# Dense stage: the next block's rows turned by VectorE in squares of 32 in place of TensorE's transposes

## The reference

```python
def _moe2_ref(x, w_in, w_out):        # x 4352 x 512, w_in 512 x 2048, w_out 2048 x 512
    h = x @ w_in
    neg = h <= -1.0
    pos = h >= 1.0
    g = np.where(pos, h, np.where(neg, 0.0, (h + 1.0) ** 2 / 4.0))
    return (g @ w_out).astype(np.float32)
```

## Time and profile before

| | |
|---|---|
| median of 3 runs | 1357.77 us (1357.71 to 1357.79) |
| the profiled execution's own time | 1359.21 us |
| its span, first to last instruction | 1357.5 us |
| mean granted TensorE clock | 0.995 |
| TensorE matmuls busy | 1333.6 us (98%) |
| VectorE busy | 776.6 us (57%) |
| ScalarE busy | 406.3 us (30%) |
| dense stage, first hidden to last result | 583.2 to 1345.2 us |

### The profile page before, as it was taken

How to read it: one execution, slowest core, us unless ns; L and a number is a source line. 1 busy time by engine, 2 the same in 40 slices (tenths; PEclk the granted TensorE clock), 3 DMA queues, 4 the chain that set the end, 5 groups by cost and what they waited for, 6 DMA issues and landing times.

```text
span 1357.5 us, 19931 instructions
## 1 busy us (share of the span) xinstructions
PE 1333.6 (98%) x6638; PEld 1116.2 (82%) x6639; DVE 776.6 (57%) x1521; ACT 406.3 (30%) x641; POOL 386.6 (28%) x213
## 2 busy tenths in 40 slices
PE   8999999999999999999999999999999999999996
PEld 6998888888888888788888888888888888888885
DVE  4677888888888888754444444444444444444342
ACT  3555222222222222322222222222222222222232
POOL 2377372775571849270010100100001001010010
PEclk9999999999999999999999999999999999999998
DMA  6656233434441525420010100100100001010000
GB/s 151 170 167 222 107 110 106 170 108 142 136 170 46 169 78 191 136 94 16 16 40 17 38 16 16 39 15 8 47 15 34 18 9 39 15 39 1 0 32 16
DMA packets 80586, 100.54 MB, mean 74 GB/s; under 512 B 46112, under 2 KB 46112, under 8 KB 80032
## 3 DMA queue, kind: packets, MB, share of 16 engines
q1 hardware_dynamic: 60160, 61.94, 14.9%
q10 hardware_dynamic: 13856, 20.19, 4.8%
q0 software_dynamic: 6528, 17.87, 3.5%
HBM read 69.80 MB, written 30.18 MB: 74 GB/s over the span
## 4 chain that ended last, share of the span: by engine, by line
PE 94%; DMA 1%; DVE 1%; issue 1%; POOL 0%; ACT 0%; ACTq 0%; SPq 0%; POOLq 0%; DVEq 0%
PE area L1685 27%; PE area L1699 27%; PE area L1635 15%; PE area L1593 14%; PE area L1403 2%; PE area L1373 2%; PE area L1527 1%; PE area L1393 1%; PE area L1671 1%; PE area L1360 1%; DMA xin<-in_x 1%; PE area L1420 1%; PE area L1427 0%; DMA st_diag<-in_state 0%; DMA slot_x<-rows,found 0%
## 5 line engine op out<-in xcount | busy, mean ns | idle before, releaser
L1699 PE MATMUL area<-W,gs 128*128 128x512 f32 x1632 | 397.4, 391 | 1.0 <-DVE gs L1267 1.0
L1685 PE MATMUL area<-ys,W 128*128 128x512 f32 (+1 forms) x1728 | 394.4, 377 | 0.0
L1685 PEld LDWEIGHTS area<-ys,W 128*128 128x128 f32 x1728 | 313.4, 188 | 61.2
L1699 PEld LDWEIGHTS area<-W,gs 128*128 128x128 f32 x1632 | 303.0, 188 | 62.7 <-DVE gs L1267 1.4
L1213 DVE STREAM_TRANSPOSE area<-hrow 32x256 f32<-32x256 f32 x592 | 269.9, 456 | 75.3 <-ACT hrow L718 66.3
L600 POOL DMA_INDIRECT out<-orow,out_row x34 | 32.7, 961 | 708.4 <-ACT orow L804 618.5
L788 ACT ACTIVATE gate<-gate,half_col 128x512 f32<-128x512 f32 (+1 forms) x144 | 100.7, 700 | 440.7 <-DVE gate L1262 439.6
L1262 DVE TENSOR_SCALAR gate<-area 128x512 f32<-128x512 f32 (+1 forms) x144 | 95.3, 662 | 224.3 <-PE area L1685 224.1
L1635 PE MATMUL area<-W,hs 128*128 (+1 forms) x912 | 218.9, 396 | 0.5 <-issue 0.3
L1593 PE MATMUL area<-W,xs 128*128 x864 | 202.0, 389 | 0.2 <-issue 0.2
L1635 PEld LDWEIGHTS area<-W,hs 128*128 128x128 f32 x912 | 169.6, 189 | 35.5 <-issue 1.1
(11 more groups left out here) (195 smaller groups left out, 799.1 us busy)
## 6 DMA issues: line engine op xcount, KB each, us to landing
stage<-in_moe_w SPq DMA_DIRECT2D x32, 1024.0 KB, 5.5
sorted_y<-ytile ACTq DMA_DIRECT2D x38, 256.0 KB, 2.1
xtile<-slot_x ACTq DMA_DIRECT2D x36, 256.0 KB, 2.7
yrow<-sorted_y SPq DMA_DIRECT2D x34, 256.0 KB, 2.6
xin<-in_x SPq DMA_DIRECT2D x60, 128.0 KB, 2.9
stage<-in_moe_w_in SPq DMA_DIRECT2D x4, 1024.0 KB, 4.9
stage<-in_moe_w_out SPq DMA_DIRECT2D x4, 1024.0 KB, 5.3
slot_x<-zero SPq DMA_DIRECT2D x9, 256.0 KB, 3.2
```

The costliest lines, as they stand in the source:

```text
L1685: last = nc.tensor.matmul(HIDDEN[n % 2][:, 0:width], wq[:, wp, :], ys[par][:, yp, k, 0:width], start=(k == 0 and wp == HI and yp == HI), s ...
L1699: last = nc.tensor.matmul(SUMS[a], gs[n % 2][:, gp, a * P:(a + 1) * P], W[:, q // 2 + 2, wp, at:at + DM], start=(n == 0 and gp == HI and w ...
```

## The change

The transposes of TensorE in the dense stage's loop go (both calls of `turn_next` in it). VectorE turns each of the 30 row tiles in 16 instructions, each four squares of 32 (32 partitions by 128 elements), from `yrow` to the same PSUM banks. They are spread over three slices n, in pairs: behind the clamp (part 0), behind the maximum (part 1) and behind the low part (part 2). For a row tile with turning slice T the pairs stand at n = T - 2 (parts 1 and 2), T - 1 (all parts) and T (all parts); `yt_made` rises at the end of n = T. `weigh` moves from behind n = T - 2 to behind the low part of n = T - 3, and `y_lo` from behind n = T to behind the clamp of n = T + 1. The turning slices of block 0 become 5, 8, 11, 14. The turning of the first four row tiles, and ScalarE's and SyncE's programs, are as before but for those slices.

```diff
-        FIRST_TURN_AT = (6, 9, 12, 14)
+        FIRST_TURN_AT = (5, 8, 11, 14)
...
+            def squares(j, k, first, end):
+
+                if first == 0:
+                    dve.wait_ge(weighted, j + 1)
+                    dve.wait_ge(ylo_done, j - 1)
+                turned = TURNED[k].rearrange("p (d s) -> p d s", d=KD)
+                for r, q in ((n // 4, n % 4) for n in range(first, end)):
+                    last = nc.vector.transpose(
+                        turned[SQ * q:SQ * (q + 1), :, SQ * r:SQ * (r + 1)],
+                        yrow[k][SQ * r:SQ * (r + 1), :].rearrange("p (d f) -> p d f", d=KD)[:, :, SQ * q:SQ * (q + 1)])
+                if end == 16:
+                    last.then_inc(yt_made, 1)
+
+            def turn_beside(i, n, part, par, turned, turn_at):
+
+                for a in range(turned):
+                    j, at = first_row(i + 1) + a, n - turn_at[a] + 2
+                    if at == 3 and part == 0:
+                        y_lo(j, 1 - par, a)
+                    if at == 0 and part > 0:
+                        squares(j, a % 2, 2 * part - 2, 2 * part)
+                    if at in (1, 2):
+                        squares(j, a % 2, 6 * at - 2 + 2 * part, 6 * at + 2 * part)
+                for a in range(turned):
+                    if part == 2 and n == turn_at[a] - 3:
+                        weigh(first_row(i + 1) + a, a % 2)
+
-            def gates(i, n, width):
+            def gates(i, n, width, par, turned=BIG, turn_at=TURN_AT):
                 h, g = HIDDEN[n % 2][:, 0:width], gate[n % 2][:, 0:width]
                 dve.wait_ge(hidden_made, K2 * i + n + 1)
                 nc.vector.tensor_scalar(g, h, -1.0, 1.0, ALU.max, ALU.min).then_inc(clamped, 1)
-
+                turn_beside(i, n, 0, par, turned, turn_at)
                 dve.wait_ge(squared, K2 * i + n + 1)
                 nc.vector.tensor_tensor(h, g, h, ALU.max).then_inc(gated, 1)
+                turn_beside(i, n, 1, par, turned, turn_at)
                 dve.wait_ge(ghi_done, K2 * i + n + 1)
                 nc.vector.tensor_tensor(gs[n % 2][:, LO, 0:width], h, gs[n % 2][:, HI, 0:width].bitcast(F32), ALU.subtract
                                         ).then_inc(glo_done, 1)
+                turn_beside(i, n, 2, par, turned, turn_at)
...
-            def turns(i, n, par, turned=BIG, turn_at=TURN_AT):
-                if n + 2 in turn_at[:turned]:
-                    a = turn_at.index(n + 2)
-                    weigh(first_row(i + 1) + a, a % 2)
-                if n in turn_at[:turned]:
-                    a = turn_at.index(n)
-                    y_lo(first_row(i + 1) + a, 1 - par, a)
...
             def block_of_rows(i, par, next_width=BIG * P):
                 for n in range(1, K2):
                     hidden(i, par, n)
-                    if n in TURN_AT[:next_width // P]:
-                        turn_next(i, TURN_AT.index(n))
                     result(i, n - 1)
...
-                if n in FIRST_TURN_AT:
-                    turn_next(0, FIRST_TURN_AT.index(n))
```

More of the change, by code:

```diff
@@ L1274, in out_copy @@
                 nc.vector.tensor_copy(orow[a][:, :], SUMS[a]).then_inc(out_copied[1], 1)
-            def turns(i, n, par, turned=BIG, turn_at=TURN_AT):
-                if n + 2 in turn_at[:turned]:
-                    a = turn_at.index(n + 2)
-                    weigh(first_row(i + 1) + a, a % 2)
-                if n in turn_at[:turned]:
-                    a = turn_at.index(n)
-                    y_lo(first_row(i + 1) + a, 1 - par, a)
             def block_of_rows(i, par, width=BIG * P, turned=BIG):
                 for n in range(1, K2):
-                    gates(i, n, width)
-                    turns(i, n, par, turned)
+                    gates(i, n, width, par, turned)
             for a in range(2):
@@ L1295, in _ @@
             h_lo(tail + 2)
[L1296 to L1299, removed]
+            for n in range(K2):
+                gates(0, n, BIG * P, 0, turn_at=FIRST_TURN_AT)
             for i in (1, 2):
-                gates(i, 0, BIG * P)
+                gates(i, 0, BIG * P, i % 2)
                 for a in (1, 3):
@@ L1307, in _ @@
                     i = 2 * m + 1 + q
-                    gates(i, 0, BIG * P)
+                    gates(i, 0, BIG * P, 1 - q)
                     for a in (1, 3):
@@ L1312, in _ @@
             for i, width, turned in ((BLOCKS - 2, BIG * P, 2), (BLOCKS - 1, 2 * P, 0)):
-                gates(i, 0, width)
+                gates(i, 0, width, i % 2, turned)
                 for a in (1, 3):
```

## The result

The changed kernel takes 1343.99 us (median of 4 runs, 1343.40 to 1344.39) against 1357.78 us for the kernel before, beside it on the same chip. The ratio is 0.9899 with a 95% interval of 0.9885 to 0.9913. That is 13.8 us less; 1343.5 was forecast. Run a second time it took 1344.03 us beside 1358.13 for the kernel before, ratio 0.9895 (0.9880 to 0.9910).

What follows compares the result with a forecast made beforehand. TensorE was taken to bound the dense stage; removing 30 turns of 0.48 us, with VectorE's added work hidden, gave 1357.77 - 14.3 = 1343.5 us. Own range 1342.8 to 1344.3, widened to 1342.6 to 1346.5 for 8 in 10.

Steps and rivals of the forecast that it cites:

- The price of a turn: Dense stage, TensorE: four transposes cost 0.48 us by distance between starts; 30 turns removed give 14.3 us.
- the two gaps belong to the two banks: Dense stage, TensorE: turns into one PSUM bank cost 0.45 us, into the other 0.50.
- The price on VectorE: Dense stage: each of 480 transposes of 32x128 takes 0.32 us; VectorE's busy time grows by 155 to about 932 us.
- The hiding: Gate chain: transpose pairs fit VectorE's waits or follow the low part; chain grows from 3.73 to about 3.8 us, costing nothing.
- the one on block 0: Block 0: the weighing comes two slices earlier, at n = 2, after 603.3 us; its row lands about 600.8, not late.
- the prediction's own sign: Dense stage: prediction wrong if TensorE waits for the low part, a transpose costs over 0.58 us, or groups exceed 2.72 us.
- A late instruction at the loop's back edge: VectorE's longer loop program waits for an instruction fetch at the jump back: 3.5 us, giving 1347.0; chance 0.05.
- VectorE becomes the bound, and the kernel slower than before: Dense stage: a transpose price over 0.61 us makes VectorE the bound; at 0.65 us 20 us lost, 1377; chance 0.02.
- The prediction's formula: At price p VectorE falls behind 16p - 8.9 us a turn; four turns, less 1.43 and 1.91, over seven and a half blocks.
- Its edges at 0.58 and 0.61 us: VectorE's transpose price: from 0.58 us TensorE waits; up to 0.61 it still gains, about 1350 us (chance 0.03); above, slower.
- the turns were free on TensorE: Dense stage: TensorE's 0.48 us a turn was only a displaced wait, so the time stays 1357.8 us; chance 0.02.

Runs made afterwards that it cites:

- Half of the turns: The changed kernel with TensorE again turning row tiles a = 1 and 3, 15 turns, and VectorE the other 15; 1351.78 us.
- The doubled turns: The kernel before, with each of TensorE's 30 dense-stage turns done twice, eight transposes in place of four; 1370.20 us.
- the doubled transposes: The changed kernel with every VectorE transpose issued a second time into a spare SBUF tile, 960 in all; 1382.80 us, ratio 1.0157.

## Why the prediction was right, and where it was not

**The price of a turn** on TensorE, 0.48 us, held: the stage without the mishap of block 0 (the run with its turning slices at 6, 9, 12, 14) is 739.2 us, 14.2 less than before, against 14.3 forecast. Half of the turns gave back 7.1 us. That it was read as a distance between starts and not as the printed 272 ns is what made it right: the printed 272 ns, read as a cost, would have given 33 us. The doubled turns put 0.42 of the 0.48 on the transposes themselves. The guess that the two gaps belong to the two banks was wrong, without effect on the sum.

**The price on VectorE**, 0.32 us, was measured as 0.322; its busy time came to 935.3 us where 932 was said, and 4.2 of that is the long weighing.

**The hiding** held at each place named: first pair free, second pair 0.06 us (0.01 to 0.05 was said), third behind the chain; 1.43 us of slack left. Outside block 0 TensorE's groups stay at 2.72 us and a block at 87.04, as was said. At the block's start 0.24 us of idle was forecast in front of the clamp, and 0.32 is shown (timeline, start of block 1):

```profile
678.09 0.48 DVE L1250 TENSOR_SCALAR yrow<-yrow,info_of 128x512 f32<-128x512 f32 x1
...
680.09 0.69 DVE L1289 TENSOR_SCALAR gate<-area 128x512 f32<-128x512 f32 x1 [0.32 <-PE area L1703]
```

**The step that failed** is the one on block 0: "`weigh` comes two slices earlier, at n = 2 [...] not late [...] GpSimd's queue is passed by nothing." I asked only whether its data had landed, and not what else was at work in SBUF at that time. The trace of the kernel before could have told it, since GpSimd's last subtraction starts there just before the 603.3 us at which the prediction puts the weighing (timeline, kernel before):

```profile
602.95 4.63 POOL L475 TENSOR_TENSOR W<-stage,W 128x2048 fp32r<-128x2048 f32 x1
```

It was moved from a free stretch into this subtraction, and cost 1.1 us. By the prediction's own sign, "wrong if TensorE waits for the low part", that place was wrong: TensorE waited for it once. In the stage this is the whole distance from the forecast, 13.2 us in place of 14.3. The median was off by less, 0.5 us, since it fell by 0.6 us more than the stage did. That lies within the interval of the ratio (11.8 to 15.6 us) and has no cause that I can show; so far the nearness of the median is luck.

**The rivals.** A late instruction at the loop's back edge did not come: TensorE waits for the low part just twice in the stage, once in block 0 and once at the very end, as before. One of the two instruction queues did fetch more. That fits VectorE's longer program, but whose queue it is was not shown (page, DMA queues: packets, MB, share; 18 packets before):

```profile
q14 instruction: 26, 0.21, 0.1%
```

That VectorE becomes the bound, and the kernel slower than before, at a price over 0.61 us fits the one price tried: at about 0.64 us the doubled transposes cost 22 us more. The size was somewhat low. The prediction's formula gives 15 us there, and 20 only at 0.65. Its edges at 0.58 and 0.61 us were not tried. That the turns were free on TensorE is refuted by two runs, the half and the doubled.

Of what was built, the changed kernel with block 0's turning slices left at 6, 9, 12, 14 has the lowest median, 1343.36 us. By its time it can't be told from the changed kernel; by its stage it is 0.9 us shorter.

## What to carry to other kernels

On an engine that never waits, price an instruction by the distance from its start to the next one's, not by its printed duration. Work moved to a less busy engine is free only where it fits the waits and the slack of the chain it is put into: 16 transposes in pairs cost nothing over two or three slices, and the same 16 in one place cost 88 us. When a VectorE operation with both ends in SBUF is moved, look at what GpSimd does at its new place, not only at whether its data are there.

## What the runs showed of the hardware that was not expected

With all transposes in one place, a wait of 1.96 us on TensorE was followed in 14 of 30 turns by some 3 us at half the clock (0.50), and a group took up to 4.47 us in place of 2.72. Behind the other waits, which were of 1.43 us, of 1.96 and, twice in block 0, of 2.06 and 2.08, the group took 2.81 to 2.89. So the length of the wait alone does not decide; what does was not tried.

A VectorE weighing of 0.48 us took 4.64 to 4.67 us when it started 0.21 to 0.24 us behind a GpSimd subtraction of 4.61 us, while transposes of VectorE from SBUF to PSUM kept their price beside the same work.
